# A three-stage attention and MLP kernel: two small operations move from VectorE to GpSimd, and P V is issued in four groups

## The reference

```python
# q, k, v: (4, 8, 576, 64)
scores = (1/8) * q @ k.T                             # per batch and head, 576 x 576
thresh = max(scores, axis=-1) - tau
scores = where(scores >= thresh, scores, -1e9)
attn   = exp(scores - max(scores))
attn   = attn / (sum(attn) + 1e-9)
x      = (attn @ v) -> (2304, 512)
h = x @ w_in;   x = (s * relu(h)**2 + b) @ w_out      # d_ff 2048
h = x @ w_in2;  y = (relu(h) + alpha * min(h, 0)) @ w_out2
```

## Time and profile before

| | us |
|---|---|
| median of 3 runs | 1149.88 (1149.6 to 1151.83) |
| the profiled execution, whole | 1150.09 |
| its span in the trace | 1148.3 |
| PE busy | 1118.0 (97%) |
| VectorE busy | 581.8 (51%) |
| ScalarE busy | 534.5 (47%) |
| GpSimd busy | 255.1 (22%) |

### The profile page before, as it was taken

One profiled execution on the slowest core, in us unless ns is written; L12 is line 12 of the kernel. 1 busy time (PEld: TensorE's weight loads), 2 busy tenths in 40 slices (PEclk: granted clock), 3 DMA queues, 4 the chain that ended last, 5 costly groups with the idle time before them and its releaser, 6 DMA issues.

```text
span 1148.3 us, 20861 instructions
## 1 busy us (share of the span) xinstructions
PE 1118.0 (97%) x6457; PEld 987.4 (86%) x6457; DVE 581.8 (51%) x1159; ACT 534.5 (47%) x1018; POOL 255.1 (22%) x440
## 2 busy tenths in 40 slices
PE   6899999999999999999999999999999999999998
PEld 5666767666669999999999999899999999999997
DVE  6788999999955432423323345532323233232322
ACT  4676777777765432323223245533434333343432
POOL 3454555555557400000000025600000000000000
PEclk9999999999999999999999999999999999999999
DMA  6555556565502200000000004300000000000000
GB/s 155 137 137 133 141 126 148 124 144 129 130 11 74 65 0 0 0 0 0 0 0 0 0 27 128 100 2 1 27 0 27 0 27 0 0 27 0 27 0 27
DMA packets 100110, 59.64 MB, mean 52 GB/s; under 512 B 67040, under 2 KB 83440, under 8 KB 100080
## 3 DMA queue, kind: packets, MB, share of 16 engines
q1 hardware_dynamic: 100080, 59.28, 20.5%
HBM read 30.94 MB, written 4.72 MB: 31 GB/s over the span
## 4 chain that ended last, share of the span: by engine, by line
PE 91%; SPq 4%; issue 2%; DMA 1%; ACT 1%; DVE 1%; ACTq 0%; DVEq 0%
PE psum L793 24%; PE psum L795 24%; PE psum L794 24%; PE psum L899 6%; PE psum L815 4%; PE psum L872 4%; PE psum L817 2%; SPq L349 2%; PE psum L801 1%; PE psum L869 1%; SPq L325 1%; PE psum L880 1%; SPq L328 1%; DMA k_low_half<-k_lo 1%; ACT pt L544 0%
## 5 line engine op out<-in xcount | busy, mean ns | idle before, releaser
L793 PE MATMUL psum<-x_hi,win_hi 128*128 128x384 f32 x768 | 259.4, 338 | 3.0 <-DVE x_raw L757 2.7
L794 PE MATMUL psum<-x_lo,win_hi 128*128 128x384 f32 x768 | 259.0, 337 | 0.0
L795 PE MATMUL psum<-x_hi,win_lo 128*128 128x384 f32 x768 | 259.0, 337 | 0.0
L793 PEld LDWEIGHTS psum<-x_hi,win_hi 128*128 128x128 f32 x768 | 143.9, 187 | 6.9 <-issue 3.0
L794 PEld LDWEIGHTS psum<-x_lo,win_hi 128*128 128x128 f32 x768 | 143.9, 187 | 3.3
L795 PEld LDWEIGHTS psum<-x_hi,win_lo 128*128 128x128 f32 x768 | 143.9, 187 | 0.0
L748 DVE SCALAR_TENSOR_TENSOR act_r<-act_n,nalpha,act_r 128x384 f32<-128x384 f32 x96 | 59.4, 619 | 160.4 <-ACT act_r L599 160.4
L738 DVE SCALAR_TENSOR_TENSOR act_r<-act_r,s_c 128x384 f32<-128x384 f32 x96 | 84.9, 884 | 109.3 <-ACT act_r L590 109.3
L593 ACT ACTIVATE g_hi<-act_r,b_c 128x384 fp32r<-128x384 f32 x96 | 59.2, 617 | 150.3 <-PE psum L795 101.0
L795 PE MATMUL psum<-g_hi,wout_lo 128*128 128x384 f32 x384 | 128.6, 335 | 0.0
L793 PE MATMUL psum<-g_hi,wout_hi 128*128 128x384 f32 x384 | 128.3, 334 | 0.0
(11 more groups left out here) (81 smaller groups left out, 1657.2 us busy)
## 6 DMA issues: line engine op xcount, KB each, us to landing
k_twice<-k_hi SPq DMA_DIRECT2D x64, 144.0 KB, 2.5
stage<-in_moe_w_out_dram SPq DMA_DIRECT2D x32, 256.0 KB, 2.6
k_low_half<-k_lo SPq DMA_DIRECT2D x32, 144.0 KB, 2.4
out_dram<-y_sb SPq DMA_DIRECT2D x18, 256.0 KB, 2.1
raw_q<-in_q_dram SPq DMA_DIRECT2D x32, 128.0 KB, 2.4
raw_k<-in_k_dram SPq DMA_DIRECT2D x32, 128.0 KB, 2.5
raw_v<-in_v_dram SPq DMA_DIRECT2D x32, 128.0 KB, 2.7
q_both<-q_hi SPq DMA_DIRECT2D x32, 128.0 KB, 2.3
```

The lines of the kernel that those rows point to most:

```text
L793: nc.tensor.matmul(dst, lhs[0], rhs[0], start=first, stop=False)
L794: nc.tensor.matmul(dst, lhs[0], rhs[1], start=False, stop=False)
L795: return nc.tensor.matmul(dst, lhs[1], rhs[0], start=False, stop=final)
```

## The change

`none_in` moves from DVE to POOL, where it is one `tensor_scalar` for each column with two pointer operands, hence nine for each pair instead of five on two columns. It stands directly ahead of `extra`, which waits for it on POOL's own semaphore. `den` moves to POOL too, at the head of the next step, ahead of `normalise` and `threshold`; it waits for `extra` and for the mask. DVE keeps `rinv`, which waits for `den`. P V of the first group of queries goes from steps 10, 11, 13, 14, 15 to steps 11 (two chunks) and 13 (three); that of the second from steps 18 (two), 19, 20, 21 to 18 (two) and 20 (three). The copy out of the first group goes from step 15 to 14.

```diff
-        PV = {10: [(0, 0)], 11: [(0, 1)], 13: [(0, 2)], 14: [(0, 3)], 15: [(0, 4)],
-              18: [(1, 0), (1, 1)], 19: [(1, 2)], 20: [(1, 3)], 21: [(1, 4)]}
+        PV = {11: [(0, 0), (0, 1)], 13: [(0, 2), (0, 3), (0, 4)],
+              18: [(1, 0), (1, 1)], 20: [(1, 2), (1, 3), (1, 4)]}
-        FIRST_OUT, SECOND_OUT = 15, 21
+        FIRST_OUT, SECOND_OUT = 14, 21
 # GpSimd
             def all_masked(t):
                 r = slice(0, P)
+                for i in range(t.cols.start, t.cols.stop):
+                    c = slice(i, i + 1)
+                    mm = nc.gpsimd.tensor_scalar(none_in[r, c], negm[r, c], tau_c[r, :], negm[r, c], ALU.add, ALU.is_lt)
+                mm.then_inc(none_ok, 1)
                 wait_alone(pool, none_ok, t.twos + 1)
                 nc.gpsimd.tensor_scalar(extra[r, t.cols], none_in[r, t.cols], float(S), 1e-9, ALU.mult,
                                         ALU.add).then_inc(extra_ok, 1)
+            def denominator(t):
+                r, c = slice(0, P), t.cols
+                wait_alone(pool, extra_ok, t.twos + 1)
+                wait(pool, freed, t.uses + 1)
+                nc.gpsimd.tensor_tensor(den[r, c], rsum[r, c], extra[r, c], ALU.add).then_inc(den_ok, 1)
             def emit(n0, l):
+                if before.tile and before.closes:
+                    denominator(before)
                 if normed_now.tile:
                     normalise(normed_now)
                 if after.tile:
                     threshold(after)
 # VectorE
-            def nothing_left(t):
-                wait_alone(dve, normed, t.count - TPP + 1)
-                wait(dve, maxed, t.count + 1)
-                nc.vector.scalar_tensor_tensor(out=none_in[r, c], in0=negm[r, c], scalar=tau_c[r, :], in1=negm[r, c],
-                                               op0=ALU.add, op1=ALU.is_lt).then_inc(none_ok, 1)
-            def denominator(t):
-                wait_alone(dve, extra_ok, t.twos + 1)
-                wait(dve, freed, t.uses + 1)
-                nc.vector.tensor_tensor(den[r, c], rsum[r, c], extra[r, c], ALU.add).then_inc(den_ok, 1)
             def invert(t):
+                wait_alone(dve, normed, t.count - TPP + 1)
                 wait(dve, den_ok, t.twos + 1)
                 nc.vector.reciprocal(rinv[r, c], den[r, c]).then_inc(rinv_ok, 1)
```

More of the change, by code:

```diff
@@ L472, in emit @@
             def emit(n0, l):
-                t, after, normed_now = Use(n0, l), Use(n0, l + 1), Use(n0, l - NORM_LAG)
+                before, t, after, normed_now = Use(n0, l - 1), Use(n0, l), Use(n0, l + 1), Use(n0, l - NORM_LAG)
+                if before.tile and before.closes:
+                    denominator(before)
                 if normed_now.tile:
@@ L674, in mask, with invert @@
                                                op0=ALU.is_ge, op1=ALU.mult, accum_out=rsum[r, t.col]).then_inc(freed, 1)
-            def nothing_left(t):
+            def invert(t):
                 r, c = slice(0, P), t.cols
                 wait_alone(dve, normed, t.count - TPP + 1)
-                wait(dve, maxed, t.count + 1)
-                nc.vector.scalar_tensor_tensor(out=none_in[r, c], in0=negm[r, c], scalar=tau_c[r, :], in1=negm[r, c],
-                                               op0=ALU.add, op1=ALU.is_lt).then_inc(none_ok, 1)
-            def denominator(t):
-                r, c = slice(0, P), t.cols
-                wait_alone(dve, extra_ok, t.twos + 1)
-                wait(dve, freed, t.uses + 1)
-                nc.vector.tensor_tensor(den[r, c], rsum[r, c], extra[r, c], ALU.add).then_inc(den_ok, 1)
-            def invert(t):
-                r, c = slice(0, P), t.cols
                 wait(dve, den_ok, t.twos + 1)
@@ L713, in emit @@
                     row_max(after)
-                if before.tile and before.closes:
-                    denominator(before)
                 if t.prepares:
@@ L719, in emit @@
                     mask(t)
-                if after.tile and after.closes:
-                    nothing_left(after)
                 if before.tile and before.closes:
```

## The result

The changed kernel takes 1155.78 us (median of 7 runs, 1152.92 to 1156.17); the kernel before, run beside it, 1150.29 (1149.6 to 1152.06). The ratio is 1.0032 with a 95% interval of 1.002 to 1.0044: slower by a third of a percent. The forecast of 1153 had the direction; the loss is somewhat larger, and it has a second source that was counted at zero.

The account below looks back on a forecast made before the run. PE was taken to bound each pair up to tile 5, the k_lo transfer with DVE's mask its end. P V 0, DVE 0, POOL +0.2 us over 15 periods gave +3 on 1150, hence 1153 us; range 1143 to 1163.

Parts of the forecast that it names:

- The bound: PE bounds only each pair's start; at its end the k_lo transfer lands at most 0.03 us ahead of DVE's mask.
- second stretch: From the fill of tile 5 to the next pair's tile 0: claimed to keep its 9.29 us, hiding 0.70 us saved.
- P V: Five groups fewer save 1.75 us of PE time a pair, but the forecast counted 0 in the period.
- first stretch: From the fill of tile 0 to that of tile 5, 10.18 us before; P V's change there forecast at 0.
- The loop over tile 3's buffer: From tile 3 to tile 5, which reuses its PSUM buffer: 3.93 us forecast, against 4.63 before.
- the way to tile 3: From tile 0 to tile 3: 6.31 us forecast against 5.80 before, plus two or three turn waits at 0.1 each.
- The bound of +0.4: Upper bound on P V's cost a pair before tile 5, if every waiting turn pays a restart of 0.27 us.
- VectorE: Losing none_in and den takes 3.6 us a pair off DVE, 17.8 to 14.2; counted as 0 in time.
- GpSimd: POOL's work grows from 10.6 to 16.7 us a pair; cost taken as +0.2 us, bounds 0 to +1.0.
- Rival 1: PE remains the bound up to tile 5, keeping 0.3 to 0.5 us a pair: 1144 us; chance 0.20.
- Rival 2: POOL becomes the bound, late thr reaching DVE, at 0.6 to 0.9 us a pair: 1161 us; chance 0.20.
- Rival 3: Nothing moves: POOL's chain stays hidden, bunching and savings cancel, 1150 us; chance 0.23.

Follow-up runs that it names:

- P V alone: Kernel before with only P V regrouped into four groups and the copy out at step 14; none_in and den stay on VectorE: 1154.17 us, ratio 1.0015.
- k first: Kernel before with ScalarE's split of k moved ahead of the exponential of tile 5 and a copy, nothing left out: 1143.78 us, ratio 0.9935.

## Why the prediction was right in direction and short in size

**The bound.** Half right. That the transfer of k_lo sets the end of the second stretch and hides what is saved there was shown (19.47 to 18.92 us once it is earlier; 9.26 and 9.30 us in stretches with two groups fewer). That DVE's mask shares in it was wrong: the prediction took the named releaser for a real condition and did not look up in the code which masks the fill waits for.

**P V.** The step that failed is "So the first stretch is worth -0.2 + 0.2 = 0". It measured +0.15 a pair, by P V alone. The loop over tile 3's buffer was sized well, 3.93 forecast and 3.89 measured. What was too small is the way to tile 3, 6.31 and "two or three such waits at 0.1": it took 6.72. One wait for a copy costs 0.36 us with its restart, not 0.1. That is about what a group costs (0.35), and why moving the chunk of step 19 gained nothing. The bound of +0.4 held it. The rule of the Trainium skill, "TensorEngine Tiling (Array Packing)", Key Properties, that a change of tiling mode drains TensorE, agrees with the same 0.33 against 0.13 in the chains after; what it would make of the time, 1.75 us a pair, did not come, because other waits take the place of the overhead.

**VectorE.** Right: 2.4 to 2.8 us fewer a pair, no gain seen. The prediction had 3.6; the records of neighbouring instructions overlap (183.99 + 0.17 and 184.08 above), which makes the busy sum smaller than the sum of the durations. No run took the work off VectorE without giving it to GpSimd.

**GpSimd.** Right in mechanism for the changed kernel, in every second pair: +0.2 forecast, +0.13 measured on top of P V. Alone this part costs 0.30, and by another path, which the prediction does not have: PE waits at the turn of tile 8 for POOL's normalisation. One of the prediction's own signs of being wrong did appear: DVE waits for POOL in every pair by more than 0.2 us (0.80 and 0.56, at `thr`). The estimates of the instructions held. Groups of POOL and DVE after, 60 to 300 us:

```profile
L464 POOL TENSOR_SCALAR none_in<-negm,tau_c 128x1 f32<-128x1 f32 x108 | 38.3, 366 | 0.0
L474 POOL TENSOR_TENSOR den<-rsum,extra 128x2 f32<-128x2 f32 x49 | 9.5, 195 | 12.8 <-POOL extra L467 12.8
L692 DVE RECIPROCAL rinv<-den 128x2 f32<-128x2 f32 x49 | 7.9, 161 | 2.8 <-POOL den L474 2.0
```

`none_in` takes 0.366 (0.34 estimated), `den` 0.195 (0.2), the waits 0.20 and 0.24 (0.2). The 2x of the Trainium skill, "GPSIMD Engine Reference", Engine selection, does not show at two columns: 0.195 us there and 0.149 on VectorE, a factor of 1.3. What the prediction did not see is the loop branch, 0.2 us once in two pairs, with which a chain that just fits becomes exposed.

**The sum.** 0.28 a pair against 0.20, over 15 periods 4.2 us against 3. The measured ratio is worth 3.7 us on 1150. That the sum is nearer than its terms is luck: P V was put 0.15 too low, and GpSimd 0.07 too high for its share beside P V.

**The rivals.** Rival 1 (PE's saving kept) is refuted by P V alone, behind the transfer and with it off the path. Rival 2 (POOL the bound at 0.6 to 0.9 a pair) came in part as a mechanism, POOL bounds the first stretch of every second pair and late thresholds reach DVE, but not at its price, since the instructions and waits stayed near the estimates. Rival 3 (all cancels) missed by the 0.28 of both parts.

## What to carry to other kernels

When a trace names the releaser of a wait on several conditions, look up in the code whether that releaser is a condition at all, and test it by moving the other one: one ACT instruction moved was worth 0.65%, more than both parts of this change together cost. Work that stands between two users of a single buffer can be free, as the chunk of step 19 was; before gathering such pieces into larger groups to save their overhead, ask what fills the gap. Small operations moved to an idle engine bring their own waits with them, here 0.2 us for each result handed on within the engine, and delay everything behind them in that engine's list: here the wait that cost most was not for a moved operation but for the normalisations behind them. Read each part's price from the gaps of the engine that bounds the time, in a kernel with that part alone.

## What the runs showed of the hardware that was not expected

A wait of GpSimd for its own last result costs 0.20 to 0.25 us, the branch at the end of its loop another 0.2, both as much as one of the small instructions (0.19). VectorE's `none_in` of two columns takes 0.63 us on average before, and all 50 from 60 to 300 us end within 0.02 us of the end of a normalisation on GpSimd. These waits were free where PE is the bound: with k first they are still there, and PE is busy for 60.00 of 60 us.

At the end of a pause of nearly 3 us TensorE's granted clock fell to 0.50 for about 3 us in the profile after (747.5 to 750.5 us) and stayed at 1.00 in the one before, with the same instructions. Half the clock over 3 us of work takes 1.5 us by estimate, which is what the MLP layers are longer.
